# An expert order that starts at batch 0's most wanted expert, and 128 of its tokens run while the others are routed

## What is computed

```python
x = attn.transpose(0, 2, 1, 3).reshape(1536, 320)
h = x @ w_in                                     # 320 x 2048
x = (np.maximum(h, 0) + np.log1p(np.exp(-np.abs(h)))) @ w_out
logits = x @ w_gate                              # 8 experts
e_idx = np.argmax(logits, axis=1)
gate_w = softmax(logits)[np.arange(N), e_idx]
eom = sigmoid(x @ w_output_gate)
for e in range(8):
    mask = e_idx == e
    h = np.maximum(x[mask] @ w1[e], 0.0)         # 320 x 1024
    out[mask] = gate_w[mask, None] * eom[mask, e, None] * (h @ w2[e])
```

## Time and profile before

| | us |
|---|---|
| median of 3 runs | 414.55 |
| lowest, highest | 413.3, 416.58 |
| the profiled execution | 416.05 |
| its span, first to last instruction | 414.3 |
| mean granted clock of PE, share of full | 0.984 |

### The profile page before, as it was taken

The page is one execution under the profiler, slowest core; times in us unless marked ns, Lnnn a source line. Parts: engine busy times, 40 slices in busy tenths (PEclk is TensorE's granted clock), DMA queues, the critical chain, the costliest instruction groups (busy, mean ns, idle before and its releaser), DMA issues.

```text
span 414.3 us, 9440 instructions
## 1 busy us (share of the span) xinstructions
PE 384.2 (93%) x2740; PEld 354.8 (86%) x2741; DVE 281.4 (68%) x503; ACT 227.6 (55%) x409; POOL 183.7 (44%) x216
## 2 busy tenths in 40 slices
PE   0899899899999999999999999899999999999983
PEld 0658788699999989999999999777988999889873
DVE  6989999667655697567766676687373267874231
ACT  6736763554546645665556555636555358875230
POOL 6313534335557476343433463035274323886221
PEclk9979999999999999999999999989999999999998
DMA  8989665344345745644222254325836119741110
GB/s 193 296 285 316 198 198 143 104 133 128 83 107 149 259 134 155 189 138 163 71 71 72 66 195 142 115 59 174 308 111 238 60 44 348 271 153 36 55 35 28
DMA packets 30513, 62.41 MB, mean 151 GB/s; under 512 B 9150, under 2 KB 20929, under 8 KB 29842
## 3 DMA queue, kind: packets, MB, share of 16 engines
q1 hardware_dynamic: 28610, 56.58, 43.5%
q0 software_dynamic: 1808, 5.31, 4.0%
q10 hardware_dynamic: 64, 0.15, 0.1%
HBM read 55.17 MB, written 5.85 MB: 147 GB/s over the span
## 4 chain that ended last, share of the span: by engine, by line
PE 59%; DMA 12%; issue 7%; SPq 7%; POOL 6%; DVE 6%; ACT 2%; DVEq 0%; POOLq 0%; ACTq 0%
PE ps L1759 4%; PE ps L1761 4%; PE ps L1760 4%; PE ps L1617 4%; PE ps L1619 4%; PE ps L1618 4%; DMA wout_t<-w_out_t 4%; PE ps L1714 3%; PE ps L1716 3%; PE ps L1715 3%; PE ps L1581 3%; PE ps L1743 3%; PE ps L1583 3%; PE ps L1582 3%; DMA win_raw<-w_in 3%
## 5 line engine op out<-in xcount | busy, mean ns | idle before, releaser
L933 ACT ACTIVATE soft<-ps 128x384 f32<-128x384 f32 x64 | 31.5, 492 | 68.2 <-PE ps L1586 66.6
L1213 DVE SCALAR_TENSOR_TENSOR gsum<-ps,soft 128x384 f32<-128x384 f32 x64 | 35.5, 557 | 47.9 <-ACT soft L941 47.8
L696 POOL TENSOR_TENSOR win_lo<-win_raw,win_hi 128x256 fp32r<-128x256 f32 x32 | 25.0, 780 | 85.3 <-DVE win_hi L1200 84.5
L1617 PE MATMUL ps<-wout_hi,ghi 128*128 128x336 f32 x192 | 61.0, 318 | 0.4 <-DVE glo L1219 0.4
L1619 PE MATMUL ps<-wout_hi,glo 128*128 128x336 f32 x192 | 60.7, 316 | 0.0
L1618 PE MATMUL ps<-wout_lo,ghi 128*128 128x336 f32 x192 | 60.6, 316 | 0.0
L1581 PE MATMUL ps<-xhi,win_hi 128*128 128x384 f32 x124 | 42.3, 341 | 1.9 <-DVE gsum L1213 1.6
L1583 PE MATMUL ps<-xhi,win_lo 128*128 128x384 f32 x124 | 41.9, 338 | 0.0
L1582 PE MATMUL ps<-xlo,win_hi 128*128 128x384 f32 x124 | 41.8, 337 | 0.0
L1759 PE MATMUL ps<-split,hthi 128*128 x120 | 38.3, 319 | 2.1 <-DVE htlo L1392 1.6
L1761 PE MATMUL ps<-split,htlo 128*128 x120 | 37.0, 308 | 0.0
(11 more groups left out here) (223 smaller groups left out, 964.6 us busy)
## 6 DMA issues: line engine op xcount, KB each, us to landing
e1raw<-w_e SPq DMA_DIRECT2D x24, 512.0 KB
e2raw<-w_e SPq DMA_DIRECT2D x16, 640.0 KB
win_raw<-w_in SPq DMA_DIRECT2D x32, 192.0 KB, 2.8
wout_raw<-w_out SPq DMA_DIRECT2D x32, 160.0 KB, 2.1
kq<-kq_t SPq DMA_DIRECT2D x16, 240.0 KB
wout_t<-w_out_t SPq DMA_DIRECT2D x3, 1024.0 KB, 14.7
og<-o_t SPq DMA_DIRECT2D x2, 1152.0 KB, 9.3
kr<-k_rows SPq DMA_DIRECT2D x8, 240.0 KB, 3.9
```

The source lines that it names most:

```text
L1213: dve.scalar_tensor_tensor(half(gsum, hf), ps[:, hf, 0:S // 2], 0.0, half(soft, hf), ALU.max, ALU.add).then_inc(g_done, 1)
L1617: pe.matmul(o, ghi[u][:, cols], wout_hi[u][:, :], start=opens, stop=False, skip_group_check=True)
```

## The change

1. Behind tile 17 DVE chooses batch 0's experts, PE counts them beside `hidden(19)`, and DVE finds the expert that batch 0 wants most. The experts are then run in cyclic order from that one (`turned_e`, `e_order`).
2. DVE gives the first 128 of its batch 0 tokens the rows of slot 0, PE makes their list beside `hidden(24)`, and POOL gathers them in tile 26. The remaining tokens are ordered from slot 1 on: `r_left` takes the place of `r_hot` in the places, and the first edge starts at 1.
3. SP loads no expert weights before `e_order` is known; it reads the expert's number from it, and puts a part behind each half of the loads from tile 22 on. Expert 2's loads stand ahead of the stores of batch 1's rows.
4. ACT's and DVE's splits of expert 0 move to tiles 24 to 29.
5. PE transposes slot 0's rows ahead of the last `second`. In the routing it makes slot 0's first product, transposes, and second product; slot 1's product follows where slot 0's was.
6. There is a twentieth slot place (`SLOTS = TT + E`), and the loop over slots starts at 1.

```diff
+            sp.wait_ge(order_known, 1)
+            expert = expert_of(0)
+            load_part(0, expert, 0)
+            half_loads(1, 3, 1)
+            load_part(0, expert, 1)
+            half_loads(1, 4, 0)
...
+            load_part(1, expert, 3)
+            half_loads(1, 7, 1)
+            load_part(1, expert, 4)
+            expert = expert_of(2)
+            load_first(2, expert)
+            load_second_weights(2, expert)
             for n in range(2):
                 sp.wait_ge(x2_act, 5 + 2 * n)
                 store_rows(NC + n * NC // 2, NC + (n + 1) * NC // 2)
```

```diff
@@ POOL
-            split_tiles(1 + 2 * KT, FT - 2)
+            split_tiles(1 + 2 * KT, FT - 3)
+            f = 2 * FT - 6
+            split_in(f + 1, 1)
+            pool.wait_ge(win_split, 2 * f + 4)
+            pool.wait_ge(fetch_ready, 1)
+            pool.wait_ge(x2_stored, 16)
+            load_rows(0, 0)
+            split_out(f, 0)
+            pool.wait_ge(xs_loaded[0], 16)
+            split_step(FT - 3, 1)
...
@@ ACT
+            tiles(FT // 2 + 1, FT - 4)
+            first = 2 * FT - 8
             act.wait_ge(e1_loaded, E1_PARTS)
             for k in range(KT):
-                softplus(2 * (first + k))
+                softplus(first + k)
                 split1_part(0, k)
-                softplus(2 * (first + k) + 1)
...
+            turn_x(0, 0)
+            last_logits()
+            last_sums(0)
+            relu_half(0, 0)
+            last_sums(1)
+            relu_half(0, 1)
+            turn_h(0)
+            act.wait_ge(logits_read, 2)
+            nc.scalar.activation(r_exp[:, :, :], r_exp[:, :, :], ACT.Exp).then_inc(route_act, 1)
+            nc.scalar.activation(r_sig[:, :, :], r_logit[:, :, E:2 * E], ACT.Sigmoid).then_inc(route_act, 1)
             split1(1, 0)
             split2(1, 0)
-            turn_x(0, 0)
             turn_x(1, 1)
-            relu(0)
+            relu(1)
+            turn_x(2, 0)
             act.wait_ge(slots_ready, 1)
```

```diff
@@ DVE
+            def expert_order():
+                most = lambda n: e_most[:, :].to_broadcast([P, n])
+                chosen = lambda n: e_first[:, :].to_broadcast([P, n])
+                chain(dve.tensor_reduce(e_total[:, :], e_count[:, 1, :, :], AX_X, ALU.add))
+                chain(dve.tensor_reduce(e_most[:, :], e_total[:, :], AX_X, ALU.max))
+                chain(dve.tensor_tensor(e_left[:, :], e_total[:, :], most(E), ALU.is_equal))
+                chain(dve.tensor_tensor(e_left[:, :], e_left[:, :], left_e[:, :], ALU.mult))
+                chain(dve.tensor_reduce(e_first[:, :], e_left[:, :], AX_X, ALU.max))
+                chain(dve.tensor_tensor(e_sum[:, :], left_e[:, :], chosen(E), ALU.add))
...
             choose(slice(0, NC), r_logit[:, 0:NC, 0:E], None)
+            tiles(9, read_1=count)
+            expert_order()
+            dve.tensor_copy(l_token[:, :, :], token_1[:, 0:NC].unsqueeze(2).to_broadcast([P, NC, 2])).then_inc(l_token_done, 1)
+            tiles(10, between=first_places)
+            first_rows()
...
+            tiles(11, between=others)
+            tiles(12, read_0=list_first)
+            split1_part(0, 0)
+            tiles(13, between=lambda: split1_part(0, 1))
+            split1_part(0, 2)
+            tiles(14)
             split2(0)
-            tiles(first + 2 + KT)
             tiles(FT - 1, last=True)
...
+            turn_h_half(0, 0)
+            dve.wait_ge(order_ready, 1)
+            holds = ps[:, 7, 0:SLOTS]
+            dve.tensor_scalar(fetch_at[:, 1:SLOTS], holds[:, 1:SLOTS], -1.0, 0.0, ALU.add, ALU.max).then_inc(fetch_ready, 1)
+            turn_h_half(0, 1)
```

```diff
@@ PE
+            def list_0():
+                pe.wait_ge(at_row_done, 1)
+                pe.wait_ge(l_token_done, 1)
+                for t in range(NC):
+                    pe.matmul(ps[:, 0, LIST_AT:LIST_AT + 2], at_row[:, t, :], l_token[:, t, :],
+                              start=(t == 0), stop=(t == NC - 1), skip_group_check=True)
...
+            turn_x(0, 0, xs_loaded[0], 16)
+            second(2 * FT - 1, 1, True)
...
+            opening_product()
+            turn_h(0)
+            keep_running(5)
+            pe.wait_ge(x2_act, 7)
+            order()
+            second_product(0, 0)
+            pe.wait_ge(put_done, 3)
+            scales(0, TT // 2)
+            turn_x(1, 1, xs_loaded[1], 16)
             scales(TT // 2, TT)
-            very_first_product()
+            next_product()
             pe.wait_ge(slots_ready, 1)
```

More of the change, by code:

```diff
@@ L168, in build_program @@
         zero_1 = keep.place("zero_1", [P, 1], F32)
-        table = keep.place("table", [P, TABLES, SLOTS + 1], I32)
+        table = keep.place("table", [P, TABLES, WIDE], I32)
         fetch_at = keep.place("fetch_at", [P, SLOTS], I32)
@@ L768, in spread, with scatter @@
                 return value[:, :].unsqueeze(2).to_broadcast([P, TT, WIDE])
[L770 to L776, removed]
+            def scatter(j, u):
                 pool.wait_ge(yout_done, j + 1)
@@ L1063, in body @@
                     when_next(act, j, sure, lambda: ahead(j, u, more2))
-                if more1 and not (isinstance(j, int) and j == 0):
+                if more1:
                     r = look_up(act, PREPARE, j, E - 1)
@@ L1212, in gate_tile @@
                     dve.wait_ge(ln_done, 2 * f + hf + 1)
+                    if hf == 0 and read is not None:
+                        read()
                     dve.scalar_tensor_tensor(half(gsum, hf), ps[:, hf, 0:S // 2], 0.0, half(soft, hf), ALU.max, ALU.add).then_inc(g_done, 1)
@@ L1219, in gate_tile, with tiles @@
                     dve.tensor_tensor(half(glo[u], hf), half(gsum, hf), half(ghi[u], hf).bitcast(F32), ALU.subtract).then_inc(glo_done, 1)
-            def tiles(i, sums_between=False, last=False):
+            def tiles(i, between=None, last=False, read_0=None, read_1=None):
                 high_in(2 * i + 1, 1, 16 * i + 16)
                 high_out(2 * i, 0, 32 * i + 32)
-                gate_tile(2 * i, 0)
-                if sums_between:
-                    sums()
+                gate_tile(2 * i, 0, read_0)
+                if between is not None:
+                    between()
                 if not last:
@@ L1257, in _ @@
                 tiles(i)
-            tiles(FT // 2, sums_between=True)
+            tiles(FT // 2, between=sums)
             def split1_part(r, k):
@@ L1577, in hidden @@
                     pe.wait_ge(g_done, 2 * f + hf + 1)
+                    if hf == 0 and beside is not None:
+                        beside()
                     cols = slice(hf * (S // 2), (hf + 1) * (S // 2))
@@ L1746, in second_product @@
             def second_product(j, u):
-                run = look_up(pe, RUN, j, E)
+                run = look_up(pe, RUN, j, E) if not isinstance(j, int) or j >= 1 else 1
                 pe.wait_ge(htlo_done, 2 * j + 1)
```

395 lines of the change are left out of this document (240 added, 155 removed).

## The result

| | before | changed |
|---|---|---|
| median of 20 runs, us | 416.56 | 413.47 |
| lowest, highest | 413.3, 418.54 | 410.03, 419.44 |
| profiled execution; its span | 416.05; 414.3 | 413.08; 411.0 |
| mean granted clock | 0.984 | 0.98 |

The ratio is 0.9931, 95% interval 0.9907 to 0.9955: 0.7% faster, 3.1 us, where 5.4 us (409.1 for 414.55) were forecast. "Faster by over 1%" was the forecast's likeliest case; the time fell within 1%. 413.47 lies inside the range (up to 413.6) by luck, for a reason that none of the cases had.

A forecast was written before the change was run, and what follows sets the result against it. PE was taken as the always busy engine, with the hole in the routing. 416.05 + 2.3 (dense stage) - 7.7 (routing) = 410.65, less 1.5 for the profiled execution: 409.1 us, range 405.2 to 413.6.

The forecast's parts named there:

- Faster by over 1%: Whole kernel: measured time below 410.4 us, chance 0.64; within 1% had 0.26, slower 0.10.
- From slot 2 on nothing changes: Slots from 2 on: no change; splits moving to slots 12 and 13 cost nothing, at most 1 us.
- The dense stage: Its end moves by 1.2 + 0.3 + 1.3 - 0.5 = +2.3 us, between +0.5 and +5.
- The wait for win_hi: Dense stage, DVE's split behind tile 29, ahead of win_hi's last cast: +1.3 us on a wait of 0.39.
- The old waits for loads: Dense stage, stretch of the old expert loads: waits of 0.3 and 0.4 us go, counted as -0.5.
- The DVE pieces: Dense stage: DVE's added instructions for experts' order, places and rows, +0.3 us for all three.
- the added matmuls and transposes: Dense stage, PE: six list matmuls, two count matmuls and three transposes of slot 0's rows, nothing hides them, +1.2 us.
- T to slot 2's product: From the dense stage's end (T) through the routing to slot 2's product: 21.65 us for 29.38, 7.7 less.
- Rival 1: Routing: the clock holds at full rate, 1.8 us less, 407.3 us; chance 0.20.
- Rivals 2, 3 and 4: Expert weights starve dense stage, 412.7 (0.20); SP's queue delays tiles, 421 (0.09); slot 0's gather lands late, 414 (0.05).
- The base: Whole kernel before: median 414.55 us, 1.5 below the profiled execution's 416.05.

The follow-up runs named there:

- e5: Changed kernel, with PE's wait for POOL's half of e2lo moved from the second product's start to ahead of its fifth k step: 409.39 us, ratio 0.9831.
- e1: Kernel before, with experts renumbered on the host to run in the changed kernel's order 6, 7, 0 to 5: 421.47 us, ratio 1.0118.
- e8: e1 plus e5's moved wait, so the kernel before in the changed order: 416.77 us, ratio 1.0018.
- e12: Kernel before with e5's moved wait alone, as a control: 415.57 us for 416.51, ratio 0.9962.
- e6: Changed kernel with both e4's and e5's edits: 407.19 us, ratio 0.9775.
- e4: Changed kernel with DVE's split of expert 0's second weights moved behind the dense stage's last gate: 410.53 us, ratio 0.9852.
- e7: Kernel before with more fillers in the routing, 16 instead of 12 and 4 instead of 2: 415.36 us for 416.45, ratio 0.9994.
- e9: e6 without its five fillers in the routing: 408.1 us, ratio 0.9826.
- e10: Kernel before without its 12 and 2 fillers around the first scale matmuls: 417.52 us for 415.39, ratio 1.0047.
- e3: Changed kernel with 20 fillers on PE in the last slot ahead of its second product: 412.99 us, ratio 0.9924.
- e2: Changed kernel with experts renumbered to run 6, 7, 0, 1, 3, 4, 5, 2, a long expert last: 411.63 us, ratio 0.9864.

## Why the prediction was wrong

**The step that failed** is "From slot 2 on nothing changes", with its price for the splits that move to slots 12 and 13: "in a slot with splits PE did not wait, so nothing, at most 1". In the slots that have a next one no product waited for a split: the cover is the next slot's first product. The last slot has none. By the forecast's own order 6, 7, 0 to 5 with its counts, expert 5 was to be alone there, its weights split one slot earlier. What hides the split was not named. The last slot measured +4.24 us in the trace. The moved wait gave back 4.1 in the medians (e5), and 4.7 in the kernel before with the same order (e1 to e8). Of the 4.24, 1.5 are the longer wait and 2.7 the clock that fell in it. The slots between, by the same sentence "nothing", took 1.53 more: the intervals of the transposes that exceed 8.44 are 9.06, 9.74, 8.88 and 8.73, for 9.25 and 8.77 before. What of that is the order's stays open (e8, e12).

**The dense stage**, forecast +2.3, measured +1.26. The wait for win_hi came to 1.78, forecast 0.39 + 1.3: right. The old waits for loads went, as forecast. The DVE pieces (expected +0.3) left no wait of PE at all. Together the waits changed by +0.7 (1.4 for win_hi, less 0.7), so under 0.6 us is left for the added matmuls and transposes, forecast +1.2; no run isolates them. In the medians the wait for win_hi costs 2.2 (e5 to e6) to 2.9 us (e4). A part of that may be the clock, which falls behind it in some executions, a price the forecast had not; the medians of four runs don't show it.

**T to slot 2's product**, forecast 29.38 to 21.65, measured 20.03. Slot 1's product, forecast at T + 14.1, came at T + 13.78, with ACT's cast of xthi behind table load and splits as forecast, but PE's own matmuls ended at the same moment. From there 7.55 was taken, with the half clock of the earlier trace rows; it took 6.25 at full clock (6.1 in e7), where the forecast gave 5.8 for that. (The order matmuls' old place, given as T + 8.0, is where they end; they start at T + 6.3 in both kernels.) Rival 1 was right for this stretch: in all eight profiles of the new routing every window from 262 to 293 is at 1.00, in e9's without the fillers too. The gain it promised (1.8) should be smaller in the median, since the kernel before did not lose the clock each time (e1, e7, e8).

Over the runs, PE's idle time bears on the clock more than one profile told. The grant fell to half in waits of 2.72 (e10, 0.2 us after its start) and 3.08 us (here, 2.4 us after its start), and stayed full in e9's routing with one of 0.7. In some executions it also fell 0.2 to 1.5 us after one of 1.78 had ended (e5, e3), 0.6 after one of 1.28 (e12), and 2.4 to 2.6 after one of 0.78 (e12). The Trainium skill's rule (TensorE: Matmul & The Clock Gate, "Why this matters for your kernels") is to avoid long idle gaps of PE between bursts of matmuls; by it the new routing keeps its clock, and the traces agree there, but they show falls behind short gaps too, of 0.78 to 1.78 us.

**Rivals 2, 3 and 4** did not happen: no wait for expert weights, none of SP's making, and the gather of slot 0, issued at 228.36, had landed long before PE's transposes of its rows at 259.4.

**The base.** The forecast took 1.5 off the profiled execution for a median of 414.55, of three runs; twenty give 416.56. So 409.1 missed 413.47 by 4.4, of which 2.0 is the base and 2.3 the change: -3.1 for -5.4. The last slot's 4.2 and the cadence's 1.5 were missing; the routing gave 1.6 more and the dense stage cost 1.0 less. So the trace's terms turn -5.4 into -2.3. The other 0.8 of the two profiled executions' difference is their attention stage, which the change doesn't touch.

**By medians**: the order alone costs 4.9 (e1), of which the moved wait gives back 4.7 (e8); the rest of the change is worth about -7.4 (e5 against e8). Taking the dense wait out as well brings another -2.2 (e6).

## What to carry to other kernels

Where a wait is hidden, name the instruction that hides it and look for the iteration that lacks it: the last one has no next iteration's work, and a change of order can put there what had slack everywhere. When two engines make the halves of an operand, wait for each half ahead of its first use, not for both ahead of the first. A stall of PE can cost more than its length, since the clock may fall in it or behind it, as in several executions here with stalls of 1.8 to 3.2 us; and a half clock read in one profiled execution is no constant to add to a sum.

## What the hardware showed unexpectedly

- After a wait of 3.1 to 3.2 us in the last slot the grant was at half for nearly the whole product of 24 matmuls (the changed kernel, e1), or fell only 1.3 us into it (e4: 0.91 in the window from 398, 0.50 in the three behind). After 1.6 us at the same place it stayed full through the product in all ten profiles that had that wait (before, e2 and e5 to e12).
- After one and the same wait of 1.77 to 1.79 us in the dense stage it fell in two profiles of four. With e3's fillers in its place (behind 0.96 us of idle) the grant stayed full where it fell with 3 us of idle.
- The gathered rows, 4.5 us from issue to landing in the changed kernel's median (3.9 before), were 0.3 to 1.8 us late for PE near slot 6 in several runs (longest 1.75, e2), while expert weights took nearly all of the bandwidth: from 322 to 334 us of e6 the DMA share was 0.95 or more in every two us, and SP's queue moved 3.89 of 4.35 MB. There the rows took 6.7 us, two gathers.
